# First batch of a fused attention and expert kernel: another order of transfers, roundings and low parts

## What is computed

```python
# 4 batches, 8 heads, 576 tokens, head size 64, model width 512
scores = scale * q @ k.T; scores = where(mask, scores, -1e9)   # heads 0-3: the last 32 keys
a = softmax(scores); x = a @ v                                 # heads 4-7: every 4th of 128 keys
xk = mu_k * x + (1 - mu_k) * x_prev; xr = mu_r * x + (1 - mu_r) * x_prev
kk = maximum(xk @ w_k, 0)                                      # 512 -> 1024
x = sigmoid(xr @ w_r) * (kk * kk @ w_v)                        # -> 512
# second part: 4 experts, each causal attention with head size 64 and an output
# projection; the two best experts of a token are mixed by a softmax of their logits
```

## Time and profile before

| | |
|---|---|
| runs | 547.62 us median (547.53 to 549.23, 3 runs) |
| the profiled execution | 548.58 us, span of the profile 546.8 us |
| PE busy in the span | 531.0 us, 97% |
| DVE, ACT, POOL busy | 61%, 49%, 42% |
| granted TensorE clock, mean | 0.994 |

### The profile page before, as it was taken

How to read it: one execution, slowest core, us unless ns; L and a number is a source line. 1 busy time by engine, 2 the same in 40 slices (tenths; PEclk the granted TensorE clock), 3 DMA queues, 4 the chain that set the end, 5 groups by cost and what they waited for, 6 DMA issues and landing times.

```text
span 546.8 us, 12317 instructions
## 1 busy us (share of the span) xinstructions
PE 531.0 (97%) x5042; PEld 474.5 (87%) x5042; DVE 335.3 (61%) x687; ACT 267.7 (49%) x692; POOL 230.0 (42%) x285
## 2 busy tenths in 40 slices
PE   7899898999999999999999999999999999999997
PEld 6789898998669999999767989999976899999765
DVE  4779959713588983930468895672247785630461
ACT  5788464223764534423484553432267463322484
POOL 7667765321354651431254554233044564230250
PEclk9899999999999999999999999999999999999999
DMA  8993110210003202201002120100000200000002
GB/s 298 341 347 96 46 40 39 78 34 1 2 24 109 63 17 78 62 18 34 2 1 88 46 78 1 34 2 1 2 2 1 86 2 1 2 1 1 1 1 88
DMA packets 8935, 29.62 MB, mean 54 GB/s; under 512 B 1200, under 2 KB 1200, under 8 KB 8880
## 3 DMA queue, kind: packets, MB, share of 16 engines
q1 hardware_dynamic: 6256, 24.12, 14.0%
q10 hardware_dynamic: 2624, 4.72, 2.7%
HBM read 24.12 MB, written 4.72 MB: 53 GB/s over the span
## 4 chain that ended last, share of the span: by engine, by line
PE 77%; ACT 7%; DVE 7%; POOL 5%; issue 1%; DMA 1%; SPq 0%; POOLq 0%; DVEq 0%; ACTq 0%
PE MM L568 21%; PE MM L570 19%; PE MM L569 19%; PE OA L556 3%; PE TR L719 2%; PE OA L742 2%; PE TR L541 2%; ACT c_prob L931 2%; PE SC L691 2%; PE SC L525 2%; POOL k_lo L1422 1%; ACT c_probT L944 1%; PE MM L691 1%; DMA raw_wr_lo<-in_w_r 1%; DVE c_negmax L1266 1%
## 5 line engine op out<-in xcount | busy, mean ns | idle before, releaser
L1422 POOL TENSOR_TENSOR k_lo<-ring,k_hi 128x288 fp32r<-128x288 f32 x64 | 55.8, 874 | 79.0 <-ACT k_hi L908 79.0
L1450 POOL TENSOR_SCALAR c_prob<-c_prob,c_inv,gates 128x512 f32<-128x512 f32 (+3 forms) x64 | 38.6, 612 | 100.3 <-DVE c_inv L1276 100.3
L568 PE MATMUL MM<-k_hi,wv_hi 128*128 128x288 f32 x256 | 76.2, 298 | 3.0 <-POOL wv_lo L1459 1.9
L568 PE MATMUL MM<-act_hi,wk_hi 128*128 128x288 f32 x256 | 77.5, 303 | 0.1
L569 PE MATMUL MM<-k_lo,wv_hi 128*128 128x288 f32 x256 | 75.5, 295 | 0.0
L569 PE MATMUL MM<-act_lo,wk_hi 128*128 128x288 f32 x256 | 75.3, 294 | 0.0
L570 PE MATMUL MM<-k_hi,wv_lo 128*128 128x288 f32 x256 | 75.3, 294 | 0.0
L570 PE MATMUL MM<-act_hi,wk_lo 128*128 128x288 f32 x256 | 75.2, 294 | 0.0
L1208 DVE RECIPROCAL gate_r<-gate_r 128x288 f32<-128x288 f32 x32 | 62.5, 1953 | 1.1
L1161 DVE SCALAR_TENSOR_TENSOR mix<-xT,one_less,mix 128x288 f32<-128x288 f32 x64 | 51.7, 811 | 8.9 <-ACT mix L1020 8.0
L568 PEld LDWEIGHTS MM<-k_hi,wv_hi 128*128 128x128 f32 x256 | 48.0, 187 | 3.9 <-POOL wv_lo L1459 2.1
(11 more groups left out here) (189 smaller groups left out, 1381.5 us busy)
## 6 DMA issues: line engine op xcount, KB each, us to landing
qkT<-in_qk SPq DMA_DIRECT2D x16, 591.5 KB, 3.8
vn<-in_v SPq DMA_DIRECT2D x16, 432.0 KB, 4.6
out_x<-c_prob ACTq DMA_DIRECT2D x16, 224.0 KB, 2.3
raw_wk_lo<-in_w_k SPq DMA_DIRECT2D x4, 512.0 KB, 16.5
raw_wv_lo<-in_w_v SPq DMA_DIRECT2D x4, 512.0 KB, 18.5
raw_wr_lo<-in_w_r SPq DMA_DIRECT2D x2, 512.0 KB, 8.2
out_x<-c_prob ACTq DMA_DIRECT2D x4, 256.0 KB, 2.0
raw_cv_lo<-in_c_v SPq DMA_DIRECT2D x1, 520.0 KB, 17.7
```

What stands on the lines that cost most here:

```text
L568: nc.tensor.matmul(dst, w2[0], x2[0], start=first, stop=False)
L1422: nc.gpsimd.tensor_tensor(lo, ring[:, ITEM[u] % RING, :], hi.bitcast(fp32), ALU.subtract)\
L1450: nc.gpsimd.tensor_scalar(prob_tile(u), prob_tile(u), c_inv[:, u:u + 1], gate, ALU.mult, ALU.mult).then_inc(c_prob, 1)
```

## The change

The order of work in the first batch is changed, and four waits are moved. No operation of the computation is added or taken away; the same products are summed in another order for the first two units v.

- SP issues the four loads of queries and keys first; the load of chunk r0 comes behind them.
- In the hand-written lists ACT begins with the exponentials (0, 1, 2) and rounds r0 behind them; DVE makes the low part of r1 (before: POOL); ACT copies the masks to the upper partitions late; k0 is the last chunk rounded there, and k1 and k2 are rounded in step 0.
- Low parts: v0 in step 2 (before 6), v2 in step 6 (8), cv in 25 (16), ck in 29 (17), cq in 29 (18), co in 33 (19). The engines stay as they were.
- In the first half of the first batch ACT rounds a squared item directly behind its square (before: one step later).
- Units v 0 and 1 of the first half run pass by pass: hi x hi for both, then the pass with the items' low parts, then the pass with the weights' low parts.
- The experts wait for each weight's low part where it is first used.

```diff
-    HI_STEP = [None] * 5 + [1, 1, 2, 4, 6, 13, 14, 15, 16]
-    LO_STEP = [None] * 3 + [2, 4, 0, 6, 5, 8, 9, 16, 17, 18, 19]
+    HI_STEP = [None] * 3 + [0, 0, 1, 1, 2, 4, 6, 13, 14, 15, 16]
+    LO_STEP = [None] * 3 + [2, 4, 0, 2, 5, 6, 9, 25, 29, 29, 33]
...
-    FIRST_PE += [(1, TURN), (2, TURN), (1, APPLY), (3, TURN), (2, APPLY), (3, APPLY), ("warm", 4)]
-    FIRST_DVE = [(0, SCORE), (1, SCORE), (0, SOFT), (2, SCORE), (1, SOFT), (2, SOFT), (3, SCORE), ("mu", 0), (3, SOFT)]
-    FIRST_DVE += [("mix", 0), ("mix", 1), ("mix", 2), ("mix", 3)]
-    FIRST_ACT = [("hi", 0), (0, EXP), (1, EXP), (2, EXP), (0, TURN), ("hi", 1), (0, APPLY), (3, EXP), (1, TURN)]
-    FIRST_ACT += [(2, TURN), (1, APPLY), ("hi", 2), (3, TURN), ("hi", 3), (2, APPLY), (3, APPLY)]
-    FIRST_ACT += [("scale", 4), ("scale", 5), ("hi", 4), ("scale", 6), ("mix_hi", 4)]
-    FIRST_POOL = [("lo", 0), (0, SOFT), (1, SOFT), (2, SOFT), ("lo", 1), (3, SOFT)]
+    FIRST_PE += [(1, TURN), (1, APPLY), (2, TURN), (3, TURN), (2, APPLY), (3, APPLY), ("warm", 4)]
+    FIRST_DVE = [(0, SCORE), (1, SCORE), (0, SOFT), (2, SCORE), (1, SOFT), (3, SCORE), ("mu", 0), (2, SOFT), (3, SOFT)]
+    FIRST_DVE += [("mix", 0), ("mix", 1), ("lo", 1), ("mix", 2), ("mix", 3)]
+    FIRST_ACT = [(0, EXP), (1, EXP), (2, EXP), ("hi", 0), (0, TURN), (3, EXP), (1, TURN), (0, APPLY), ("hi", 1)]
+    FIRST_ACT += [(1, APPLY), (2, TURN), (3, TURN), (2, APPLY), (3, APPLY)]
+    FIRST_ACT += [("scale", 4), ("hi", 2), ("scale", 5), ("masks", 0), ("scale", 6), ("mix_hi", 4)]
+    FIRST_POOL = [(0, SOFT), (1, SOFT), ("lo", 0), (2, SOFT), (3, SOFT)]
...
             load_qk(sp, 0, 1)
-            load_chunk(sp, 0)
             load_qk(sp, 0, 2)
             load_qk(sp, 0, 3)
+            load_chunk(sp, 0)
...
+                if (b, half) == (0, 0):
+                    rest = range(FT - 2, FT)
+                    phases = {0: [(m, early, x) for x in range(3) for m in range(2)] + [(0, rest, x) for x in range(3)],
+                              1: [(1, rest, x) for x in range(3)]}
+                    for m, items, phase in phases.get(n, []):
...
+                            if phase == 0:
+                                pe.wait_ge(chunk_hi, V_CHUNK + f // (FT // 4) + 1)
+                                pe.wait_ge(item_hi, f + 1)
+                                nc.tensor.matmul(dst, w_hi, x_hi, start=f == 0, stop=False)
+                            elif phase == 1:
+                                pe.wait_ge(item_lo, f + 1 + RING)
+                                nc.tensor.matmul(dst, w_hi, x_lo, start=False, stop=False)
+                            else:
+                                pe.wait_ge(chunk_lo["v", f // (FT // 4)], 1)
+                                last = nc.tensor.matmul(dst, w_lo, x_hi, start=False, stop=f == FT - 1)
...
                         nc.scalar.activation(slot, slot, ACT.Square).then_inc(squared, 1)
+                        act_item_hi(act_, b, u)
```

More of the change, by code:

```diff
@@ L593, in pe_dense @@
                 parts = {0: [(0, early), (1, early), (0, range(FT - 2, FT))], 1: [(1, range(FT - 2, FT))]}
+                if (b, half) == (0, 0):
[3 more added lines that the diff above has]
+                    for m, items, phase in phases.get(n, []):
+                        dst = (pe_mm_bank(pe, b, u - n + m) if 0 in items and phase == 0 else
+                               bank(MM, (u - n + m) % 2))[:, 0:HALF]
+                        for f in items:
+                            w_hi, w_lo = [t[:, f, m * 128:(m + 1) * 128] for t in wv2]
+                            x_hi, x_lo = [t[:, f * HALF:(f + 1) * HALF] for t in k2]
+                            if phase == 0:
[8 more added lines that the diff above has]
+                                last = nc.tensor.matmul(dst, w_lo, x_hi, start=False, stop=f == FT - 1)
+                    if n in phases:
+                        last.then_inc(mm_full, 1)
+                        return
                 for m, items in parts.get(n, [(n, range(0, FT))]):
@@ L596, in pe_dense @@
                     for f in items:
-                        if half == 0 and (n, m) == (0, 0) and f % (FT // 4) == 0:
-                            pe.wait_ge(chunk_lo["v", f // (FT // 4)], 1)
                         if (n, m) == (0, 0):
@@ L757, in pe_experts @@
         def pe_experts(pe, b, ahead):
-            for what in ("cv", "ck", "cq", "co"):
-                pe.wait_ge(chunk_lo[what, 0], 1)
             for what, n in PROJECTIONS:
+                if (what, n) == ("kq", 0):
+                    pe.wait_ge(chunk_lo["ck", 0], 1)
+                    pe.wait_ge(chunk_lo["cq", 0], 1)
+                if (what, n) == ("v", 0):
+                    pe.wait_ge(chunk_lo["cv", 0], 1)
                 dst = pe_mm_bank(pe, b, mm_index(what, n))
@@ L802, in pe_experts @@
             pe_attend(pe, b, PAIR_TILES - 1)
+            pe.wait_ge(chunk_lo["co", 0], 1)
             for n in range(NT):
@@ L1041, in act_batch @@
                     act_attention(act_, b + 1, i, TURN)
-                act_item_hi(act_, b, i - 1)
+                if not (0 < i <= B_UNITS and UNIT[i - 1][1] == "k" and squared_by_act(b, i - 1)):
+                    act_item_hi(act_, b, i - 1)
                 if ahead:
@@ L1077, in _ @@
                     act_chunk(act_, o)
-                    if o == 0:
-                        act_.wait_ge(const_ready, 2)
-                        nc.scalar.activation(ident2_up, ident2, ACT.Copy).then_inc(upper_ready, 1)
-                        nc.scalar.activation(band_up[:, IN_BANK:TA, :], band[:, IN_BANK:TA, :], ACT.Copy)\
-                            .then_inc(upper_ready, 1)
+                elif p == "masks":
+                    act_.wait_ge(const_ready, 2)
+                    nc.scalar.activation(ident2_up, ident2, ACT.Copy).then_inc(upper_ready, 1)
+                    nc.scalar.activation(band_up[:, IN_BANK:TA, :], band[:, IN_BANK:TA, :], ACT.Copy)\
+                        .then_inc(upper_ready, 1)
                 elif p == "scale":
```

1 line of the change is left out of this document (added).

## The result

The changed kernel takes 546.74 us (median of 14 runs, 546.31 to 548.31); the kernel before, run beside it, takes 549.49 us (14 runs, 547.38 to 551.08). The ratio is 0.9959, with a 95% interval from 0.9946 to 0.9973: 0.4% faster, 2.2 us (the two medians lie 2.75 us apart, because the ratio is not taken from them). The profiled executions differ by 2.02 us: 546.56 against 548.58.

The account below looks back on a forecast made before the run. PE, busy 97% of the span, was taken as the bound, with DVE, POOL and ACT close behind from 34 to 64 us. 1.3 + 1.2 = 2.5 us off 548.58 gave 546.1, median 545.1; 8-in-10 range 543.0 to 547.0.

Parts of the forecast that it names:

- first term of the sum: Start and first units v, up to unit 14: 1.3 us earlier, bounds 0.7 and 2.0, limited by DVE's backlog.
- the zero for ck: Start of the experts: ck's low part ready about 0.3 us before needed; lateness would cost below 1 us; nothing counted.
- The median of the runs shown is 1.0 lower, so 545.1 there: From the forecast profiled execution of 546.1 us to the median of runs: 1.0 lower, 545.1 us, 0.5% faster.
- step 4: PE's 1.5 us stall at 89.9 us: 1.2 us earlier, 0.3 left, bounds 0.9 and 1.5.
- the slow stretch of the clock goes, or shrinks: Rival, start: small products at 1.2 GHz speed up, 1.1 us more, 3.6 us in all, 544.0; chance 0.09.
- It is absorbed: Rival: ACT later at unit 4 or DVE's backlog unchanged; 0 to 1.4 us gained, 546.9 in the middle; chance 0.19.
- Step 1: Start: earlier exponentials and scores bring the first row of the dense part 1.7 us earlier, bounds 1.0 and 2.2.
- Step 2: First unit k (unit 4): ACT's `gate_r` leaves 0.6 of 1.7 us, bounds 0 and 1.1; new PE wait about 1.3 us.
- Step 3: First units v: the 1.9 us wait goes, DVE's backlog limits the gain to 1.3 us; `ring` wait about 1.2 us.
- the open price: DVE's durations in the first batch: the same subtraction took 2.31 us at 39.49 and 1.16 at 43.13.
- a rival with a gain: DVE keeps up, all stalls go, DVE's backlog ending some 1.5 us earlier still: 543.8 us; chance 0.17.
- Step 5: Masks, experts' waits, rounding behind the square: in-step rounding removes ACT's ring waits where DVE is the bound, worth nothing.

Follow-up runs that it names:

- e8_zeros: The kernel before with 7 products of zeros ahead of PE's wait for v2's low part: 548.27 us, ratio 0.9985.
- e2_v: The kernel before with only the units v changed: new order of passes, low parts of v0 and v2 in steps 2 and 6: 548.98 us, 0.9990.
- e3_experts: The kernel before with only the low parts of cv, ck, cq, co in steps 25, 29, 29, 33 and the experts' waits moved: 548.68 us, 0.9989.
- e4_before: The kernel before, unchanged, run as one more kernel: 549.36 us, ratio 0.9998; its profile 549.63 us.
- e5_ck_first: The changed kernel with ck's low part in step 25 and cv's in step 29: 546.02 us, ratio 0.9947.
- e10_hi_later: The changed kernel with low parts of ck, cv in steps 25, 29, v0, v2 in 6, 8, and v0, v1 rounded one step later: 545.95 us.
- e6_v_lo_old: The changed kernel with the low parts of v0 and v2 back in steps 6 and 8, new order of passes kept: 545.96 us, ratio 0.9941.
- e7_no_square: The changed kernel with each squared item again rounded one step later: 547.45 us, ratio 0.9978.
- e1_start: The kernel before with only the start changed (load order, hand-written lists, k1's and k2's roundings, masks): 548.42 us, ratio 0.9985.

## Why the prediction was off

Most places were right. What failed is the way from the trace to the median, the size of the first term of the sum for a kernel before at full clock, and the zero for ck.

- **"The median of the runs shown is 1.0 lower, so 545.1 there": this step failed.** The sum against the profiled execution gave 546.1. The profile after has 546.56 and the median of 14 executions is 546.74: there is no 1.0 between them. The 1.0 came from three executions of the kernel before; its median of 14 is 549.49, which is 0.9 above the profile, not below. The 547.62 is what the kernel before takes at full clock (547.65, 7 of 69 executions).
- **The term 1.3 for the start and the units v.** Against the profile before, the changed kernel is 1.10 us earlier at 72 us, near the forecast. But other profiles of the old start are ahead of that profile too: by 0.40 to 0.94 at the first unit k with a recorded clock of 1.00, and by 1.30 in e8_zeros. Against them the 1.10 is between -0.2 and 0.7. At full clock the whole change is worth 1.0 where 2.5 was forecast, and step 4 with ck is 1.35 - 0.50 = 0.85 of it, so the first term is worth about 0.2. The rest of the 2.02 between the profiles is how late the profile before happened to be (548.58 - 547.65 = 0.9). Part of that can be its stretch at half clock, part the landing of transfers. The forecast counted neither, so that 2.02 is near 2.5 is in part luck; and so is that the medians of 14 differ by 2.75, since more than half of that goes with falls of the clock that the forecast knew nothing of.
- **One profile was taken for the kernel.** Of 69 executions only 7 had a full clock, and a second profile put the fall at 60 us, behind the wait for `wv_lo`. The rival "the slow stretch of the clock goes, or shrinks" had 0.09; its first half came true, and it priced the start only. Of the rivals "It is absorbed" (0.19, 546.9 in the middle) came nearest, in its price and at full clock also in what is left: step 4 and little more.
- **Step 1.** Forecast 1.7, bounds 1.0 and 2.2. The row that stood at 31.37 starts at 29.20: 2.2. But kernels with the old start and a clock of 1.00 there (e2_v, e3_experts, e4_before) are earlier than the profile before as well, by 0.35 to 0.94 in the first column, against 1.64 to 2.41 for the new start (without e5_ck_first, whose clock fell there). So 0.7 to 2.1, in the middle 1.4, belongs to the order by these, and as little as 0.3 beside e8_zeros (1.30); the rest belongs to the clock and to the landing of transfers. ACT's exponential came at 8.85 (forecast 8.5), the scores of pair 2 at 8.97 (8.5), those of pair 3 at 13.25 (12.7).
- **Step 2.** The wait is there: 0.93 us (forecast 1.3), unit 4 at 37.93 (38.4). The profile names nobody for it, but `gate_r` of unit 2 starts at 37.43 (37.8) and ends 0.1 us ahead of unit 4, and with one rounding less in front of it (e10_hi_later) the wait is gone. 1.09 is kept where I forecast 0.6, against the profile before; against the profiles of the old start with a recorded clock of 1.00 there it is 0.15 to 0.7, and e8_zeros is even 0.2 earlier. And e10_hi_later shows that this bank was not what counts: the transposes near 46 are.
- **Step 3, "its work in that stretch is the same as before": wrong, with a small net.** DVE was given the same instructions there, and one took 1.30 us instead of 0.17, until POOL's subtraction of v0 beside it had ended. POOL's softmax product was late by that, PE waited 1.0 at 45.5, and 0.8 of the 1.09 was gone there; without v0's low part in that place (e6_v_lo_old) PE is 1.13 earlier. The rest came as forecast, because DVE had the slack: the wait for `ring` is 1.41 long (forecast 1.2), DVE's backlog ends at 63.46 instead of 63.87, and its 0.70 of slack with the 0.41 makes 1.11; measured -1.10, forecast -1.3. I had called DVE's durations the open price and had looked only for the gain.
- **The exclusion rule.** The Trainium skill (SBUF, section "Who interferes with whom") says that a DVE instruction with two SBUF inputs and a GpSimd instruction that reads SBUF keep each other out. The rows agree for the pairs of subtractions. DVE's ends 1.1 us behind POOL's, whether it took 3.07 or 2.31, and unhindered it takes 1.16. POOL's next one, at 39.26, met DVE's, which ended at 40.38; it took 3.39 instead of 2.38 and ended 2.3 us behind that. I used the rule for a rival with a gain; it cut the other way, since the change set a pair side by side that had not met before. The operation that cost the time has one input of 128x9. The same section says that a DVE instruction with at most one SBUF input does not contend outside the two-port modes, and that `tensor_scalar` can enter such a mode. The trace agrees with that in the end times (42.68 us, POOL's subtraction 42.65); in which mode it ran no run here shows.
- **Step 4.** 0.15 of the stall is left (forecast 0.3): 1.35 won. "I count nothing" for ck was wrong by 0.50 (e3_experts 0.53, e5_ck_first none).
- **Step 5, in-step rounding "nothing":** 0.4 us between the transposes near 46 and 72 us, by e7_no_square. In the new order of passes the high parts are wanted first, and without it they bind (1.1 for `k_hi`) instead of DVE.
- The sum against the profile: 1.1 at 72 us for 1.3, 1.35 for 1.2 at 89.9, less 0.5 at ck, gives 1.95; measured 548.58 - 546.56 = 2.02.

## What to carry to other kernels

Ask of a profile whether it is the kernel's usual execution: compare the recorded clock and time of many runs before a sum is laid over one of them, and do not carry the distance between one profile and a median of three over to another kernel. Behind a stall of PE the clock may fall, and then it costs more than its length; one that can't be removed may be filled with zeros (0.15% here, hardly clear of noise). When work is moved between engines that are nearly full, look at which instruction now runs beside which: the moved one costs its own time and holds up its neighbours. And try each entry of such a table by itself: altering two of them (e5, e6) found another 1.2 us in the trace, 1.6 in the medians.

## What the runs showed of the hardware

- The granted clock went to 1.2 GHz right behind a wait of 1.9 us in the middle of dense work in some executions and not in others (0.60 and 0.54 in 60 to 64 us in one profile of the kernel before, 1.00 in another), and cost 1.5 us. With seven products of zeros in the wait 5 of 12 executions had a full clock; with the old start and the wait empty, 8 of 93 had. Kernels without that wait have falls too, from 1 of 14 to 5 of 12 executions; three with one of 1.6 or 1.7 us at nearly the same place had falls in 2 of 18. In the profile of e5_ck_first one lies between 24 and 28 us (0.62), where PE had been busy for 2.45 of the 4 us before. Which waits bring it on, and why only sometimes, stays open.
- Groups of products took as long as at 1.2 GHz while the recorded clock was 1.00 (e2_v up to 12.6 us: 1.85 us for 36 products, else 1.03).
- A DVE operation on 128x9 numbers took 1.30 us instead of 0.17 when it met a subtraction of a chunk on POOL, and ended with it (e2_v and the changed kernel). In e1_start and e6_v_lo_old, where POOL has no subtraction at that time, it took 0.17.
- A subtraction of a chunk took 1.16 us on DVE and 2.38 on POOL where nothing held it up. Where DVE's started during POOL's it ended 1.1 us behind it (3.07 or 2.31 us long); where POOL's started during DVE's it ended 2.3 us behind that one (3.39 us long).
